# Hand-written orders for the first and the last groups of a three-stage mixer, four softmax parts, unchained loads and unread transposes

## What is computed

```python
w = softmax(weight_gen)                     # (2, 4160, 8 heads, 7 taps), over the taps
a[s] = sum over k of w[s, :, k] * x[s - 6 + k]          # a causal 7-tap mix, per head
xk = mu_k * a + (1 - mu_k) * a_prev;  xr = mu_r * a + (1 - mu_r) * a_prev
y  = sigmoid(xr @ w_r) * (relu(xk @ w_k) ** 2 @ w_v)    # 192 -> 1024 -> 192
h  = relu(y @ w_in)                                     # 192 -> 1024
c  = conv_w[0] * h_prev + conv_w[1] * h + conv_w[2] * h_next
out = (h * sigmoid(c)) @ w_out                          # 1024 -> 192
```

## Time and profile before

| | us |
|---|---|
| median of 3 runs | 733.61 (732.49 to 733.97) |
| the profiled execution, its own time | 733.41 |
| the profiled execution, its span | 731.6 |
| mean granted TensorE clock over the span | 0.995 |

### The profile page before, as it was taken

The page is one execution under the profiler, slowest core; times in us unless marked ns, Lnnn a source line. Parts: engine busy times, 40 slices in busy tenths (PEclk is TensorE's granted clock), DMA queues, the critical chain, the costliest instruction groups (busy, mean ns, idle before and its releaser), DMA issues.

```text
span 731.6 us, 10747 instructions
## 1 busy us (share of the span) xinstructions
PE 691.2 (94%) x3513; PEld 594.1 (81%) x3513; DVE 681.3 (93%) x1057; ACT 637.4 (87%) x1351; POOL 3.1 (0%) x8
## 2 busy tenths in 40 slices
PE   0678999999999999999999999999999999999995
PEld 0668888888888888888888888888888888888994
DVE  7889999999999999999989999999989899886786
ACT  3897999998979998897979998897979899797984
POOL 1000000000000000000000000000000000000000
PEclk9999999999999999999999999999999999999999
DMA  5611101020100102020100202020100201000000
GB/s 160 202 34 55 56 1 65 1 72 0 61 17 7 69 1 77 0 76 1 54 22 1 76 1 76 1 77 0 49 28 0 77 1 66 0 23 1 22 22 23
DMA packets 9357, 28.83 MB, mean 39 GB/s; under 512 B 1342, under 2 KB 4440, under 8 KB 9174
## 3 DMA queue, kind: packets, MB, share of 16 engines
q1 hardware_dynamic: 9144, 28.12, 11.5%
q10 hardware_dynamic: 158, 0.03, 0.0%
HBM read 21.75 MB, written 6.39 MB: 38 GB/s over the span
## 4 chain that ended last, share of the span: by engine, by line
PE 88%; DVE 5%; ACT 2%; issue 2%; DMA 1%; SPq 0%; DVEq 0%; ACTq 0%
PE up L320 39%; PE od L426 23%; PE dn L387 5%; PE dn L403 4%; PE dn L410 4%; PE dn L407 4%; PE dn L406 4%; PE dn L409 3%; PE mid L291 2%; DVE att L815 1%; DMA xin<-in_x 1%; DVE prod L803 1%; DVE cv L911 1%; DVE gat L930 1%; PE dn L405 0%
## 5 line engine op out<-in xcount | busy, mean ns | idle before, releaser
L426 PE MATMUL od<-wo_sb,gat 128*128 128x192 f32 x1040 | 187.4, 328 | 5.4 <-DVE gat L930 4.5
L426 PEld LDWEIGHTS od<-wo_sb,gat 128*128 128x128 f32 x1040 | 172.5, 191 | 12.2 <-issue 3.7
L879 DVE TENSOR_TENSOR kq_lo<-ksq,kq_hi 128x512 fp32r<-128x512 f32 (+2 forms) x144 | 91.1, 635 | 12.8 <-ACT kq_hi L553 12.6
L911 DVE SCALAR_TENSOR_TENSOR cv<-h,prm,cv 128x512 f32<-128x512 f32 (+2 forms) x144 | 98.9, 696 | 3.7 <-ACT cv L587 2.6
L587 ACT ACTIVATE cv<-h,prm 128x512 f32<-128x512 f32 (+2 forms) x144 | 97.5, 678 | 4.3 <-DVE gat L930 3.8
L921 DVE SCALAR_TENSOR_TENSOR cv<-h,prm,cv 128x512 f32<-128x512 f32 (+2 forms) x144 | 100.2, 696 | 0.9
L815 DVE TENSOR_TENSOR att<-att,prod 128x768 f32<-128x768 f32 (+2 forms) x108 | 95.7, 886 | 0.0
L803 DVE TENSOR_TENSOR prod<-xin,wgt 128x768 f32<-128x768 f32 (+2 forms) x108 | 95.5, 885 | 0.1
L578 ACT ACTIVATE h<-up 128x512 f32<-128x512 f32 (+2 forms) x144 | 78.9, 548 | 15.6 <-PE up L320 15.3
L930 DVE TENSOR_TENSOR gat<-h,cv 128x512 f32<-128x512 f32 (+2 forms) x144 | 91.1, 634 | 1.4 <-ACT cv L594 0.9
L594 ACT ACTIVATE cv<-cv 128x512 f32<-128x512 f32 (+2 forms) x144 | 84.3, 586 | 4.8 <-DVE cv L921 4.3
(11 more groups left out here) (108 smaller groups left out, 1349.3 us busy)
## 6 DMA issues: line engine op xcount, KB each, us to landing
xin<-in_x SPq DMA_DIRECT2D x14, 960.0 KB, 4.7
out<-o_sb SPq DMA_DIRECT2D x14, 384.0 KB, 2.3
wgt<-in_weight_gen SPq DMA_DIRECT2D x1, 1288.0 KB, 6.1
h<-in_moe_w_v SPq DMA_DIRECT2D x1, 768.0 KB, 4.5
wo_sb<-in_moe_w_out SPq DMA_DIRECT2D x1, 768.0 KB, 7.9
xin<-in_x SPq DMA_DIRECT2D x1, 768.0 KB, 4.1
h<-in_moe_w_k SPq DMA_DIRECT2D x1, 512.0 KB, 4.7
h<-in_moe_w_k SPq DMA_DIRECT2D x2, 256.0 KB, 5.4
```

The costliest lines, as they stand in the source:

```text
L426: mm = nc.tensor.matmul(o, lhs, wo_sb[:, c, :], start=(c == 0 and b % 2 == 0), stop=(c == NC - 1), skip_group_check=(b % 2 == 1))
L879: nc.vector.tensor_tensor(ring(kq_lo, c, n), ring(ksq, c, n), ring(kq_hi, c, n).bitcast(F32), ALU.subtract).then_inc(kql_ok, 1)
L911: nc.vector.scalar_tensor_tensor(o, win(w, c, -1), prm[:, 3 + c:4 + c], o, ALU.mult, ALU.add)\
```

## The change

**Order.** Each engine now has three lists: `first_steps` (about a hundred to three hundred calls written out), `step(i)` for i from 3 to 12, and `last_steps`, which runs from group NG - 6 to window NG. All three differ from the order of before. The middle order has the same calls, in another sequence: on PE, for example, `r_part(i, 1)` and `r_part(i, 2)` now stand among the first chunks of `up1(i)`, and `down2(i - 1, 5)` among `up2(i)`. How far ahead the mix is made is the same: `att_mult(i + 3)` still stands beside `k_lo(i + 2)`.

**Ends.** Window 17 now has three slots (its two and slot 64), and window NG only slot 0. The copies across runs go from DVE to ACT, as `wrap_after` and `wrap_before`, each in two halves of four chunks, and the memsets from DVE to POOL. `carry` of window 17 is gone. Window NG's `first_tap` needs only group 0's h, kept since the start. **Softmax** has parts of 8, 12, 20 and 26 slots. **Loads:** three waits of SP are gone. **Transposes:** PE makes 40 transposes of the identity matrix, which nothing reads, after the transpose of the parameters, and 8 more after group 0's transposes.

```diff
-        SM_ENDS = [0, FIRST[3] + 1, FIRST[6] + 1, FIRST[9] + 1, FIRST[13] + 1, TPP + 1]
+        SM_ENDS = [0, FIRST[3] + 1, FIRST[6] + 1, FIRST[11] + 1, TPP + 1]
...
+        def win_slots(w):
+            return 1 if eq(w, NG) else size(w) + (1 if eq(w, NG - 1) else 0)
...
             sp.dma_start(xin[:, (TAPS + S0) * D:XSLOTS * D], x_rows[:, S0 * D:EDGE * D]).then_inc(x2_in, 16)
-            sp.wait_ge(x2_in, 16)
             sp.dma_start(raw_wv, w_v.rearrange("(c p) n -> p c n", p=P)).then_inc(wv_in, 16)
-            sp.wait_ge(wv_in, 16)
             load_up_weights(sp, w_in, 2, wi_in)
-            sp.wait_ge(wi_in, 48)
...
+                pool.wait_ge(h_free, NC * n_windows(NG - 1) - (HALF if n == 0 else 0))
+                nc.gpsimd.memset(h3[:, half, AFTER + PPB - 1:AFTER + P:PPB], 0.0).then_inc(wrap_fix, 1)
...
+                pool.wait_ge(tap, NC * n_windows(NG - 1) + (n + 1) * HALF)
+                nc.gpsimd.memset(h3[:, half, AHEAD:AHEAD + P:PPB], 0.0).then_inc(wrap_fix, 1)
...
+            def first_steps():
+                t_part(0, 1)
+                t_part(0, 2)
+                warm(8)
+                up1(0, 0)
+                up1(0, 1)
+                up1(0, 2)
+                r_part(0, 1)
...
+            def last_steps():
...
+                down2(NG - 2, 5)
+                up2(NG - 1, 0)
+                up2(NG - 1, 1)
+                up2(NG - 1, 2)
+                up2(NG - 1, 3)
+                up2(NG - 1, 4)
+                down2(NG - 2, 6)
+                down2(NG - 2, 7)
+                up2(NG - 1, 5)
...
+            def warm(n):
+                for _ in range(n):
+                    nc.tensor.transpose(od[0][:, 0:P], ident[:, :], ident[:, :])
...
+            warm(40)
+            first_steps()
+            for i in range(3, NG - 5):
+                step(i)
+            last_steps()
...
+            def wrap_after(n):
+                half = slice(n * HALF, (n + 1) * HALF)
+                act.wait_ge(h_keep, NC)
+                act.wait_ge(h_free, NC * n_windows(NG - 1) - (HALF if n == 0 else 0))
+                nc.scalar.activation(part_of(half, AFTER, 0), part_of(half, ALONE, 1), ACT.Copy).then_inc(h_wrap, 1)
+            def wrap_before(n):
+                half = slice(n * HALF, (n + 1) * HALF)
+                act.wait_ge(h_ok, NC * (NG - 1) + (n + 1) * HALF)
+                act.wait_ge(tap, NC * n_windows(NG - 1) + (n + 1) * HALF)
+                nc.scalar.activation(part_of(half, AHEAD, 1), part_of(half, AFTER - P, 0), ACT.Copy).then_inc(h_last, 1)
...
             def conv_before(w, c, last=False):
...
+                if eq(w, NG):
+                    dve.wait_ge(h_last, c // HALF + 1)
+                    dve.wait_ge(wrap_fix, c // HALF + 3)
...
             def conv_after(w, c, last=False):
...
+                if eq(w, NG - 1):
+                    dve.wait_ge(h_wrap, c // HALF + 1)
+                    dve.wait_ge(wrap_fix, c // HALF + 1)
...
-            dve.wait_ge(h_free, NC * n_windows(NG))
-            dve.wait_ge(h_keep, NC)
-            nc.vector.tensor_copy(h3[:, :, 2 * P:3 * P - 1], h3[:, :, KEEP + P + 1:KEEP + 2 * P]).then_inc(h_wrap, 1)
-            nc.vector.tensor_copy(h3[:, :, KEEP + 1:KEEP + P], h3[:, :, P:2 * P - 1]).then_inc(h_wrap, 1)
-            dve.wait_ge(h_wrap, 2)
-            nc.vector.memset(h3[:, :, 2 * P + PPB - 1:3 * P:PPB], 0.0).then_inc(wrap_fix, 1)
-            nc.vector.memset(h3[:, :, KEEP:KEEP + P:PPB], 0.0).then_inc(wrap_fix, 1)
-            dve.wait_ge(wrap_fix, 2)
-            for s in range(NC + 1):
-                if s < NC:
-                    conv_before(NG, s, last=True)
-                    conv_after(NG, s, last=True)
-                if s >= 1:
-                    gate(NG, s - 1, last=True)
```

More of the change, by code:

```diff
@@ L417, in down2 @@
                     pe.wait_ge(wo_in, 16)
-                if c == 0 and not eq(w, 1):
+                if c == 0 and not eq(w, 1) and not eq(w, NG):
                     pe.wait_ge(o_ok, 2 * n_windows(w))
@@ new lines, in first_steps @@
+            def first_steps():
[6 more added lines that the diff above has]
+                r_part(0, 1)
+                up1(0, 3)
+                up1(0, 4)
+                r_part(0, 2)
+                down1(0, 0)
+                down1(0, 1)
+                up1(0, 5)
+                up1(0, 6)
+                up1(0, 7)
+                down1(0, 2)
+                down1(0, 3)
+                down1(0, 4)
+                t_part(1, 1)
+                t_part(1, 2)
+                down1(0, 5)
+                down1(0, 6)
+                down1(0, 7)
+                up2(0, 0)
+                up2(0, 1)
+                up2(0, 2)
+                up2(0, 3)
+                up2(0, 4)
+                up2(0, 5)
+                up2(0, 6)
+                up2(0, 7)
+                up1(1, 0)
+                up1(1, 1)
+                r_part(1, 1)
+                up1(1, 2)
+                r_part(1, 2)
+                up1(1, 3)
+                up1(1, 4)
+                down1(1, 0)
+                up1(1, 5)
+                down1(1, 1)
+                up1(1, 6)
+                down1(1, 2)
+                down1(1, 3)
+                up1(1, 7)
+                down1(1, 4)
+                t_part(2, 1)
+                down1(1, 5)
+                t_part(2, 2)
+                down1(1, 6)
+                down1(1, 7)
+                up2(1, 0)
+                up2(1, 1)
+                up2(1, 2)
+                up2(1, 3)
+                up2(1, 4)
+                up2(1, 5)
+                up2(1, 6)
+                up2(1, 7)
+                up1(2, 0)
+                up1(2, 1)
+                r_part(2, 1)
+                up1(2, 2)
+                r_part(2, 2)
+                up1(2, 3)
+                up1(2, 4)
+                down1(2, 0)
+                up1(2, 5)
+                down1(2, 1)
+                up1(2, 6)
+                down1(2, 2)
+                down1(2, 3)
+                up1(2, 7)
+                down1(2, 4)
+                down2(1, 0)
+                t_part(3, 1)
+                down1(2, 5)
+                t_part(3, 2)
+                down1(2, 6)
+                down1(2, 7)
+                down2(1, 1)
+                down2(1, 2)
+                down2(1, 3)
+                down2(1, 4)
+                up2(2, 0)
+                up2(2, 1)
+                up2(2, 2)
+                down2(1, 5)
+                up2(2, 3)
+                up2(2, 4)
@@ new lines, in step @@
+            def step(i):
+                up2(i - 1, 5)
+                up2(i - 1, 6)
+                up2(i - 1, 7)
+                down2(i - 2, 6)
+                up1(i, 0)
+                up1(i, 1)
+                r_part(i, 1)
+                up1(i, 2)
+                r_part(i, 2)
+                up1(i, 3)
+                down2(i - 2, 7)
+                up1(i, 4)
+                down1(i, 0)
+                up1(i, 5)
+                down1(i, 1)
+                up1(i, 6)
+                down1(i, 2)
+                down1(i, 3)
+                up1(i, 7)
+                down1(i, 4)
+                down2(i - 1, 0)
+                t_part(i + 1, 1)
+                down1(i, 5)
+                t_part(i + 1, 2)
+                down1(i, 6)
+                down1(i, 7)
+                down2(i - 1, 1)
+                down2(i - 1, 2)
+                down2(i - 1, 3)
+                down2(i - 1, 4)
+                up2(i, 0)
+                up2(i, 1)
+                up2(i, 2)
+                down2(i - 1, 5)
+                up2(i, 3)
+                up2(i, 4)
```

1613 lines of the change are left out of this document (1390 added, 223 removed).

## The result

| | before | after |
|---|---|---|
| median of 20 runs each | 733.09 (731.97 to 733.97) | 732.0 (731.08 to 732.8) |
| ratio, 95% interval | | 0.9984 (0.9978 to 0.999) |
| span of the profiled execution | 731.6 | 729.9 |

What follows compares the result with a forecast made beforehand. PE was taken to bound the middle, DVE the head and the changed tail. Tail 3.9, head 3.0, softmax -1.1 and transposes 0.5 gave 6.3 us off 733.4: 727.1 us; 8-in-10 range 721.5 to 732.

Steps and rivals of the forecast that it cites:

- term 1: Tail: woven last windows make it run at DVE's pace; 3.9 us gained, bounds 0.7 and 5.2.
- term 2: Head: the new order removes DVE idle time from 30 to 70 us; 3 us gained, bounds 0 and 4.9.
- rival (c): Middle: the new order stalls PE, one 1.1 us stall in each of 13 steps, 741 us; chance 0.1.
- unchained loads give nothing: Head, up to the first y_mult: it comes within half a microsecond of its 41.73, despite the earlier w_v.
- term 3: Softmax: part 2 grows from 12 to 20 slots, bringing DVE work earlier; 1.1 us lost, bounds 0 and 2.3.
- the part that is dropped saves in the middle, where PE covers both: nothing: Softmax: one part fewer saves about 1 us of DVE and a pair of table loads, without effect on the time.
- term 4: Head: unread transposes raise PE's clock level for the first matmuls; 0.5 us gained, bounds 0 and 2.6.
- rival (d): Head: the transposes leave the clock level where it is, PE idling about 3 us before up1(0, 0); 727.6 us, chance 0.17.
- the 48 transposes stand where PE idles otherwise: Head: the unread transposes take only idle PE time, beside a gain of 0.5 us.
- (a): Only the tail gains; DVE stays as late in the head and the softmax costs 1.1 us: 730.6 us, chance 0.2.
- period test of (c): Middle: a period over 42 us between sigmoid starts would show PE stalls; 41.5 us would show the forecast right.
- (b): Head more PE's than it looks: all DVE idle time goes, PE's 2.6 us count in full; 721.3 us, chance 0.15.

Runs made afterwards that it cites:

- x1_parts5: The kernel after with the five softmax parts of before, all else kept: 731.28 us, ratio 0.9977.
- y2_loads: x3_tail with the three waits of SP in the loads taken out, nothing else: 728.2 us, ratio 0.9928.
- x3_tail: Before's order of head and middle, its loads and five parts, no unread transposes; of the change only the new ends: 727.91 us, ratio 0.9932.
- w1_a_noparts: The kernel after with softmax parts from the third on cut to one slot, a copy for their exponential: 727.48 us, ratio 0.9929.
- w3_t_noparts: x3_tail with softmax parts from the third on cut to one slot, a copy for their exponential: 726.5 us, ratio 0.9909.
- y1_midold: The kernel after with before's step order in the middle, between its own first and last lists: 743.1 us, ratio 1.0135.
- w4_warm: x3_tail with 40 unread transposes at the start and 32 ahead of group 0's first tap matmul: 727.11 us, ratio 0.9921.
- y4_warm: x3_tail with 40 unread transposes at the start and 28 behind group 0's first tap matmul, ahead of the first up1: 731.33 us, ratio 0.9971.

## Why the prediction was wrong, step by step

The steps from the kernel before to the kernel after, in the order in which the runs allow them: the tail -5.15, the loads +0.3, the new order with five parts +3.1 (x1_parts5 less y2_loads, the unread transposes in it), four parts for five +0.7. Together they are -1.05; a chain of differences must close, so that is no proof of the single steps, and +0.3 and +0.7 are within the noise. Against the forecast: 5.15 gained for 3.9 in the tail, 3.4 lost for 3.0 gained by the head and the new order, 0.7 lost for 1.1 by the parts, nothing for 0.5 by the transposes. The 6.4 us of the second step are the miss.

**The tail, term 1: right, its size a little low.** 3.9 us forecast with bounds of 0.7 and 5.2; 5.15 measured by x3_tail. The 128-column chunk, which had no row, takes 0.27 + 0.27 + 0.20 by the distances of starts above, just as estimated. In x3_tail `up2(17, 0)` ends at 703.1, the last gate 19.5 us behind that, and the span 3.9 later, for 703.7, 20.3 and 3.7 in the forecast: the 1.2 us by which the term was low are 0.6 ahead of the stretch that DVE paces and 0.8 in it, less 0.2 behind it. The kernel after has the same 19.5 and 3.9 (from 706.5 on).

**The head, term 2: wrong, and the largest share of the miss.** The step "from 30 to 70 us DVE idles for 4.9 us; I take 3" assumed that a new order shortens waits. DVE idles for 5.5 us there now, and its waits for ACT's `kq_hi`, 2.6 us in two before (both of them from 30 to 70 us), are longer (waits of DVE from 30 to 70 us in the kernel after: total, times, longest):

```profile
DVE kq_lo L1774 <- ACT kq_hi L873: 3.8, 4, 1.9
```

What was won by 90 us (0.9 in the ledger) was gone at 110. The kernel without later parts tells the same: the new order's lead of 1.3 us at 90 is 0.3 at 110, while the old order, without the parts, holds 0.4 and 0.7. In the kernel after and in x3_tail DVE idles for less than 0.2 us in each 10 us from 80 to 190. The lead goes in short waits of PE for DVE. From 90 to 110 us the distances between PE's starts add up to 2.5 us more than its work in the kernel after and in w1_a_noparts, and to 1.4 in x3_tail and w3_t_noparts. The longest of them in the new order stand ahead of operands that DVE has just split (timeline of PE in the kernel after), while x3_tail has no wait for `xk_s` there:

```profile
94.26 0.45 PE L338 MATMUL up<-y_lo,wi_hi 128*128 128x384 f32 x1 [0.21 <-DVE y_lo L1794]
...
104.55 0.47 PE L338 MATMUL up<-xk_s,wk_hi 128*128 128x512 f32 x1 [0.35 <-DVE xk_s L1754]
```

So the term took DVE's idle time as what an order can win, and left out that the same order can make PE wait for DVE elsewhere. Of the 3.4 us by which the new order with five parts is slower, 1.0 is there without the later parts (by the medians); the other 2.4 are the parts' price in this order, rival (c). The step "unchained loads give nothing" was right: w_v's cast starts at 20.95 in the kernel after, the first `y_mult` at 41.38, and y2_loads gains nothing.

**Softmax, term 3: the sign right, two steps wrong.** "I take half, 1.1 us, since these groups run just ahead of the stretch that PE fills" counted on cover that was not there. The part does not run ahead of that stretch but in it: DVE makes its front at 110.35 and its back from 148.57 to 152.7, and in the kernel before PE is busy for 20.00 of 20 us from 110 to 130 already. Under the order of before, for which the rows were read, 20 slots for 12 cost 2.8 us (the ledger at 300 us), over the bound of 2.3, and the whole step from five parts to four 5.3. And "the part that is dropped saves in the middle, where PE covers both: nothing" looked at the dropped part and not at the one of 26 slots that takes its place. Rival (c) put its two halves at 3 us each; the front is 3.3 and the back 5.1. PE at 100% is not cover for a burst on DVE: the burst of 5.1 us delays a `kq_lo`, and PE stands. In the new order, the one in which it was made, the same step costs 0.7, within the bounds. That is luck: this order already pays for every part by a wait for `h`, and has one part fewer to pay for.

**Transposes, term 4: nothing where 0.5 was taken.** Both halves of the argument meet in the trace (windows of the kernel after, over the stretches of its clock, and its PE timeline):

```profile
14.60:21.40 6.80, 3.58 (x30) 3.02 (x28) 6.76 (x16) 3.06 (x7) 0.00 (x0) 1.00 0.82 273
21.50:28.20 6.70, 5.23 (x23) 5.06 (x24) 6.00 (x12) 5.14 (x16) 0.00 (x0) 0.50 1.03 333
28.40:41.80 13.40, 9.84 (x72) 8.50 (x70) 12.61 (x27) 12.38 (x29) 0.00 (x0) 1.00 0.16 49
42.00:48.70 6.70, 5.88 (x25) 5.61 (x25) 5.59 (x13) 4.98 (x15) 0.00 (x0) 0.50 0.00 0
```

```profile
9.11 7.25 PE L785 MATMUL od<-ident 128*128 128x128 f32 x40
...
22.97 0.55 PE L338 MATMUL up<-xk_hi,wk_hi 128*128 128x256 f32 x1 [3.74 <-ACT xk_hi L819]
23.32 0.41 PE L338 MATMUL up<-xk_hi,wk_lo 128*128 128x256 f32 x1
```

The transposes did bring the higher level: some 25 of the 40 start 0.21 us apart, the last 13 0.11. But PE then stood idle for 3.74 us and the first true matmuls ran at the lower level, 0.21 us apart, the time of rival (d), though not its condition that the level stays where it is. The step that failed is "the 48 transposes stand where PE idles otherwise": they do, but end 3.7 us before the first true matmul. The rule of the Trainium skill cited in the prediction ("TensorE: Matmul & The Clock Gate", Part 4: PE-mode transpose) gave the right size of the term, nothing, for another reason: here transposes alone raised the level, and the measurement decides.

**The rivals.** (a), only the tail gains, came nearest with 730.6, and its sign is there: group 5's sigmoid is not before 185, though the sigmoid's new place in the list makes that a weak test. What it lacked was (c), a middle order that stalls PE, which was priced at one stall in every step and given 0.1. The stalls are real but come only in the steps with a softmax part (`h` at 140.59 and again 0.85 us at 348.70). (a) with these two waits gives 730.6 + 1.1 + 0.85 = 732.6; that this is near 732.0 is luck in part, since its tail is 1.25 us short. The period test of (c) was too coarse for it: 41.6 us against 41.5. (b) failed at its condition: DVE's idle time in the head did not go. The range's upper end, 732.0, is just where the median lies.

**Still open:** which call of the new lists makes PE wait for DVE's splits between 90 and 110 us, since no run moved one, and what before's middle would give behind the new head, since y1_midold's seam covers it.

## What to carry to other kernels

Price a side task (here a softmax part) in every order it is to run in, and by its longest unbroken stretch on each engine. The prices of two edits do not add up: the new order alone costs 3.4 us and the larger parts alone 5.3, both together 4.1. An engine at 100% does not cover a burst on the engine that feeds it. How long a burst passes unseen depends on the place: in before's order 2.7 and 3.7 us of DVE passed without a wait of PE, 4.1 us made it wait 0.48 and 5.1 us 1.30; in the new order 2.6 us made it wait 0.59. And when both ends and the middle of a kernel are rewritten together, run an end alone: here the tail gives more than the whole gain, and with five parts before's order of the rest was the better one.

## What the hardware showed beyond what was expected

Unread transposes alone raise TensorE's clock level: in w4_warm they start at 9.02 us and the granted clock rises at 12.5, in the kernel after they start at 9.11 and it rises at 14.6. In w4_warm 32 of them take 3.66 us at the higher level, 0.11 us each; at the lower they start 0.21 apart. The place of such a filler decides: 32 ahead of a wait cost nothing that can be told (w4_warm), 28 behind it 3.4 us (y4_warm). The lower level need not cost anything: the kernel before has it from 719.4 to 722.8 us too (granted clock 0.53), and its gates start 1.25 us apart there as behind it. A pair of table loads and the exponential between them is 3.3 us of ScalarE for 12 slots and 3.7 for 20, of which the loads are 2.56 in both.
